# Scores of both heads made in two row groups, a ring of 30 score tiles, and the last two head pairs tested in groups of three tiles

## The reference

```python
scores = scale * np.matmul(q, k.transpose(0, 1, 3, 2))          # (2, 8, 576, 576), head_dim 64
kth = np.partition(scores, -top_k, axis=-1)[..., -top_k:-top_k + 1]   # top_k = 32
scores = np.where(scores >= kth, scores, -1000000000.0)
attn = softmax of scores along the last axis
x = np.matmul(attn, v), heads side by side                      # (1152, 512)
logits = x @ w_gate                                             # 8 experts, each token to its best
# each expert takes up to 288 tokens in order: y = relu(x @ w1[e]) @ w2[e]
out[token] = gate_w[token] * y                                  # dropped tokens stay 0
```

## Time and profile before

| | us |
|---|---|
| median of 3 runs | 535.17 (533.93 to 536.7) |
| the profiled execution, its own time | 540.3 |
| its span, first to last instruction | 538.3 |
| busy in the span: TensorE | 464.0 |
| VectorE | 308.2 |
| ScalarE | 243.7 |
| POOL | 235.8 |

### The profile page before, as it was taken

How to read it: one execution, slowest core, us unless ns; L and a number is a source line. 1 busy time by engine, 2 the same in 40 slices (tenths; PEclk the granted TensorE clock), 3 DMA queues, 4 the chain that set the end, 5 groups by cost and what they waited for, 6 DMA issues and landing times.

```text
span 538.3 us, 9099 instructions
## 1 busy us (share of the span) xinstructions
PE 464.0 (86%) x2901; PEld 390.8 (73%) x2901; DVE 308.2 (57%) x1521; ACT 243.7 (45%) x419; POOL 235.8 (44%) x197
## 2 busy tenths in 40 slices
PE   3999798899879998899797998009999999999993
PEld 2565476677656776677686886009999999999992
DVE  1699999799998999989985331300111111222222
ACT  1333685588855878567475582002131211322220
POOL 3333886587776767777756362300020210210222
PEclk9999998799987999979699698557999999999998
DMA  4111020110267240000010002479976766787400
GB/s 103 39 37 44 1 47 1 28 40 2 67 187 191 45 177 23 2 20 5 1 23 1 1 2 88 135 233 333 304 239 218 261 226 214 246 292 255 144 17 11
DMA packets 52310, 57.89 MB, mean 108 GB/s; under 512 B 33055, under 2 KB 33055, under 8 KB 52257
## 3 DMA queue, kind: packets, MB, share of 16 engines
q1 hardware_dynamic: 49984, 52.50, 31.7%
q0 software_dynamic: 2272, 4.73, 2.6%
HBM read 45.39 MB, written 14.18 MB: 111 GB/s over the span
## 4 chain that ended last, share of the span: by engine, by line
PE 38%; POOL 4%; issue 3%; DMA 3%; DVE 2%; ACT 1%; DVEq 0%; SPq 0%; POOLq 0%; ACTq 0%
PE ps_s L601 14%; PE ps_s L616 13%; PE ps_o L495 4%; PE ps_o L583 2%; PE ps_t L573 2%; PE ps_t L466 2%; POOL probs L374 2%; DMA dispatched<-x,r_slot 2%; POOL rest L369 1%; PE ps_s L506 1%; DMA scores<-dispatched 1%; PE ps_s L522 1%; POOL out_dram L407 0%; POOL dispatched L382 0%; DMA bad_row<-bad 0%
## 5 line engine op out<-in xcount | busy, mean ns | idle before, releaser
L374 POOL TENSOR_TENSOR probs<-scores,probs 128x576 f32<-128x576 f32 x72 | 101.4, 1414 | 60.8 <-ACT probs L678 58.9
L495 PE MATMUL ps_o<-v_aug,pT 128*128 128x128 f32 (+5 forms) x800 | 126.5, 300 | 0.0
L369 POOL TENSOR_TENSOR rest<-below,scores 128x576 f32<-128x576 f32 x72 | 99.9, 1408 | 55.7 <-DVE below L837 55.7
L495 PEld LDWEIGHTS ps_o<-v_aug,pT 128*128 128x128 f32 (+3 forms) x800 | 107.2, 195 | 14.5 <-issue 7.9
L449 PE MATMUL ps_s<-kT,qT 64*128 64x288 f32 x256 | 94.2, 520 | 3.5 <-ACT scores L653 2.8
L407 POOL DMA_INDIRECT out_dram<-yo,numbers x24 | 22.0, 915 | 163.5 <-DVE yo L1017 162.9
L779 DVE MAX8 cand<-scores 128x8 f32<-128x96 f32 x432 | 72.7, 240 | 17.4 <-ACT scores L653 14.9
L601 PE MATMUL ps_s<-scores,w_sb 128*128 128x192 f32 (+4 forms) x512 | 78.6, 309 | 0.6 <-ACT scores L731 0.6
L466 PE MATMUL ps_t<-ident,probs 128*128 128x128 f32 (+1 forms) x360 | 60.4, 303 | 19.7 <-ACT pT L691 15.8
L601 PEld LDWEIGHTS ps_s<-scores,w_sb 128*128 128x128 f32 x512 | 74.7, 194 | 0.9 <-ACT scores L731 0.9
L616 PE MATMUL ps_s<-scores,w_sb 128*128 128x192 f32 (+4 forms) x512 | 74.5, 304 | 0.0
(11 more groups left out here) (100 smaller groups left out, 332.4 us busy)
## 6 DMA issues: line engine op xcount, KB each, us to landing
w_sb<-in_moe_w_dram SPq DMA_DIRECT2D x16, 2048.0 KB, 9.8
dispatched<-empty SPq DMA_DIRECT2D x18, 257.0 KB, 6.3
scores<-dispatched SPq DMA_DIRECT2D x24, 192.8 KB, 3.0
out_dram<-empty SPq DMA_DIRECT2D x9, 256.0 KB, 3.1
q_nat<-in_q_dram SPq DMA_DIRECT2D x16, 128.0 KB, 2.3
k_nat<-in_k_dram SPq DMA_DIRECT2D x16, 128.0 KB, 2.4
v_aug<-in_v_dram SPq DMA_DIRECT2D x16, 128.0 KB, 2.4
out_dram<-yo,numbers POOLq DMA_INDIRECT x24, 3.4
```

The source lines that it names most:

```text
L369: nc.gpsimd.tensor_tensor(rest[:, n % 3, :], below[:, n % 3, :], score_tile(n), ALU.mult).then_inc(rest_ready, 1)
L374: nc.gpsimd.tensor_tensor(probs[:, n % PROBS, :], score_tile(n), probs[:, n % PROBS, :], ALU.subtract).then_inc(masked_ready, 1)
L495: last = nc.tensor.matmul(dst, lhs, v_aug[0:keys, g % 2, c, h, 0:width], start=(c == 0), stop=(c == TT - 1))
```

## The change

TensorE makes the scores of the two heads of a pair together, row by row (`qk_heads`): the matmuls of head 0 and head 1 alternate, head 0 into `ps_s[:, 0]` and head 1 into `ps_s[:, 1]`; the tail tile is made last (`qk_tail`). `made_at` and `tile_made` turn the order of the search into the order of making and back. The ring has 30 tiles, LEAD is 22, and w1 lies in the memory of the ring. The last two pairs are tested after every three tiles (12 tests), POOL's masks come closer from group 19 on, and the last tests stand elsewhere among VectorE's last groups. The steps of the router's work are new, and the second batch's logits have a place of their own in PSUM.

```diff
-    LEAD = 18
-    HELD = 21
-    ROUTED = [0, 2, 4, 6, 10, 12, 16]
+    LEAD = 22
+    HELD = 30
+    ROUTED = [0, 2, 4, 6, 8, 16, 19]
+    CHOSEN = 18
+    PAIRWISE = PAIRS - 2
+    CHECKS = PAIRWISE + 3 * (PAIRS - PAIRWISE)
+    ENDING = 3 * PAIRWISE
...
-        w1_sb = sb("w1_sb", [P, 2, CH, F])
...
+        w1_sb = carve(2 * CH * F).rearrange("p (u c f) -> p u c f", u=2, c=CH)
...
+        def made_at(n):
+            g, t = divmod(n, TILES)
+            return TILES * g + (2 * t if t < FULL else 2 * (t - FULL) - 1 if t > FULL else TILES - 1)
+        def tile_made(k):
+            g, e = divmod(k, TILES)
+            return TILES * g + (FULL if e == TILES - 1 else e // 2 + e % 2 * (FULL + 1))
+        def check_of(n):
+            return n // TILES if n < TILES * PAIRWISE else PAIRWISE + n // 3 - ENDING
...
-            gather_bad(6)
+            for i in range(PAIRWISE, CHECKS - 1):
+                gather_bad(i)
             load_v(7)
-            gather_bad(7)
+            gather_bad(CHECKS - 1)
...
+            masked = 0
             for m in range(GROUPS + 3):
                 if m < GROUPS:
                     push_down(3 * m)
                     push_down(3 * m + 1)
                 if m < GROUPS and m % 3 == 0:
                     push_down(3 * m + 2)
-                if m >= 3:
-                    mask(3 * (m - 3))
-                if m < GROUPS and m % 3 != 0:
+                due = 3 * (m - 2) if m <= ENDING + 2 else min(ALL, 3 * ENDING + 4 * (m - ENDING - 2))
+                if m == GROUPS + 2:
+                    due = ALL
+                for n in range(masked, due):
+                    mask(n)
+                    if n == masked and m < GROUPS and m % 3 != 0:
+                        push_down(3 * m + 2)
+                if masked >= due and m < GROUPS and m % 3 != 0:
                     push_down(3 * m + 2)
-                if m >= 3:
-                    mask(3 * (m - 3) + 1)
-                    mask(3 * (m - 3) + 2)
+                masked = max(masked, due)
...
-            def qk(n):
-                g, t = divmod(n, TILES)
-                if t == 0:
+            def qk_heads(g, r):
+                if r == 0:
                     pe.wait_ge(nat_copied, 2 * (g + 1))
-                if n >= 2:
-                    pe.wait_ge(s_ready, n - 1)
+                if g + r > 0:
+                    pe.wait_ge(s_ready, TILES * g + 2 * r)
                 for half in range(2):
                     keys = slice(half * HALF, (half + 1) * HALF)
-                    dst = ps_s[:, n % 2, half, 0:HALF]
-                    if t != FULL:
-                        h, r = (0, t) if t < FULL else (1, t - FULL - 1)
-                        last = nc.tensor.matmul(dst, qT[h * D:(h + 1) * D, g % 2, r * P:(r + 1) * P],
+                    for h in range(2):
+                        last = nc.tensor.matmul(ps_s[:, h, half, 0:HALF], qT[h * D:(h + 1) * D, g % 2, r * P:(r + 1) * P],
                                                 kT[h * D:(h + 1) * D, g % 2, keys], start=True, stop=True)
-                    else:
-                        for h in range(2):
-                            last = nc.tensor.matmul(dst[h * TAIL:(h + 1) * TAIL, :],
-                                                    qT[h * D:(h + 1) * D, g % 2, FULL * P:S],
-                                                    kT[h * D:(h + 1) * D, g % 2, keys], start=True, stop=True)
+                        if half == 1:
+                            last.then_inc(s_in_psum, 1)
...
-                    qk(s)
+                    if s % TILES == TILES - 1:
+                        qk_tail(s // TILES)
+                    elif s % TILES % 2 == 0:
+                        qk_heads(s // TILES, s % TILES // 2)
...
-                if s == ALL + ROUTED[CH] + 1:
+                if s == ALL + CHOSEN:
...
-            def copy_scores(n):
-                act.wait_ge(s_in_psum, n + 1)
+            def copy_scores(k):
+                n = tile_made(k)
+                act.wait_ge(s_in_psum, k + 1)
                 if n >= HELD:
                     act.wait_ge(masked_ready, n - HELD + 1)
+                slot = 0 if k % TILES == TILES - 1 else k % TILES % 2
                 nc.scalar.activation(score_tile(n).rearrange("p (h s) -> p h s", h=2),
-                                     ps_s[:, n % 2, :, 0:HALF], ACT.Copy, scale=SCALE).then_inc(s_ready, 1)
+                                     ps_s[:, slot, :, 0:HALF], ACT.Copy, scale=SCALE).then_inc(s_ready, 1)
...
-            def edges(g):
-                act.wait_ge(thr_checked, g + 1)
-                if g >= 2:
+            def edges(i, g, tiles):
+                act.wait_ge(thr_checked, i + 1)
+                if g >= 2 and tiles.start == 0:
                     act.wait_ge(exp_ready, TILES * (g - 1))
-                nc.scalar.activation(edge[:, g % 2, :], thr[:, g % 2, :], ACT.Copy, scale=BIG).then_inc(edges_ready, 1)
-                nc.scalar.activation(nmax[:, g % 2, :], tops[:, g % 2, :, 0], ACT.Copy, scale=-1.0).then_inc(edges_ready, 1)
+                nc.scalar.activation(edge[:, g % 2, tiles], thr[:, g % 2, tiles], ACT.Copy, scale=BIG).then_inc(edges_ready, 1)
+                nc.scalar.activation(nmax[:, g % 2, tiles], tops[:, g % 2, tiles, 0], ACT.Copy, scale=-1.0).then_inc(edges_ready, 1)
             def excess(n):
                 g, t = divmod(n, TILES)
-                if t == 0:
-                    edges(g)
-                    act.wait_ge(edges_ready, 2 * (g + 1))
+                i = check_of(n)
+                if t == 0 or i != check_of(n - 1):
+                    edges(i, g, slice(0, TILES) if g < PAIRWISE else slice(t, t + 3))
+                    act.wait_ge(edges_ready, 2 * (i + 1))
...
-                    dve.wait_ge(s_ready, n + 1)
+                    dve.wait_ge(s_ready, made_at(n) + 1)
                     after(bounded[j])
                     for c in range(SEGS):
                         part = score_tile(n)[:, c * (S // SEGS):(c + 1) * (S // SEGS)]
                         last = add(nc.vector.max(cand[:, j, c * 8:c * 8 + 8], part))
                     found.append(last)
-                    if m % 3 == 1 and m > 3 and j == 0:
-                        counted = count_bad(m // 3 - 1)
-                    if m % 3 == 1 and m > 3 and j == 1:
-                        recheck(m // 3 - 1, counted)
+                    for i in range(CHECKS):
+                        if m == (3 * i + 4 if i < PAIRWISE else i - PAIRWISE + ENDING + 2):
+                            if j == 0:
+                                counted = count_bad(i)
+                            if j == 1:
+                                recheck(i, counted)
...
+            def tiles_of(i):
+                return (i, slice(0, TILES)) if i < PAIRWISE else (i // 3 + PAIRWISE * 2 // 3, slice(i % 3 * 3, i % 3 * 3 + 3))
...
+                if m == GROUPS:
+                    recheck(CHECKS - 2, count_bad(CHECKS - 2))
                 if m > 0:
                     search_rest(m - 1)
                     pick(m - 1)
-                if m > 0 and m % 3 == 0:
+                if m > 0 and m % 3 == 0 and m <= ENDING:
                     find_bad(m // 3 - 1)
+                if m > ENDING:
+                    find_bad(m - 1 - ENDING + PAIRWISE)
                 if m < GROUPS:
                     mark_below(m)
-            recheck(PAIRS - 1, count_bad(PAIRS - 1))
+            normalise(PAIRS - 2, 0)
+            recheck(CHECKS - 1, count_bad(CHECKS - 1))
             dve.wait_ge(consts_ready, 11)
-            normalise(PAIRS - 2, 0)
             choose_experts(0)
             normalise(PAIRS - 2, 1)
             assign_slots(0)
```

44 lines of the change are left out of this document (27 added, 17 removed).

## The result

The change made the kernel **slower by 1.4%**: 542.23 us, the median of 14 runs (539.49 to 545.35), against 535.6 for the kernel before, run beside it on the same chip (14 runs, 529.53 to 542.52). The ratio is 1.014, 95% interval 1.0107 to 1.0172. The ratios leave out executions over 1.5% above the fastest of their kernel (4 of the kernel before here, none of the changed one); by the medians of all it is 1.2%, and the ratios of the first four experiments lie 0.4 to 0.9% above those of their medians, mostly for the same reason. I had forecast 525.7 us, a range of 516 to 534, and faster with a chance of 0.81: the time lies outside the range, and it moved the other way.

A forecast was written before the change was run, and what follows sets the result against it. It took VectorE to pace the search, with TensorE working off a late tail and then the experts. Terms 5.5 - 2.0 + 1.6 + 1.0 - 15.6 = -9.5 us, from the 535.17 median, gave 525.7 us, range 516 to 534.

The forecast's parts named there:

- start, third group of tiles: At the start, pairs of tiles wait for both score copies; VectorE's third group at 41.0 against 35.48: +5.5 us, nothing absorbs it.
- wait for the row of counts: On SP's queue, the last pair's v load behind one more gather lands before its first user: nothing.
- more tests: On VectorE, 12 tests instead of 8, about 0.4 us each: +1.6 us for four.
- `picked`: In the last groups, POOL's masks sit next to `picked` more often, up to two more collisions: +1.0 us, bounds 0 and 2.8.
- tail: After E, the last test frees three tiles instead of nine; attention ends at E + 32.2 instead of E + 47.8: -15.6 us.
- LEAD and HELD: In the search, VectorE's first three waits for weighted values stay, the fourth, 2.03 us, goes: -2.0 us.
- fourth rival: TensorE goes cold behind every test; normalisation waits after all seven, +11.4, slow tail +5.1: +7, 542 us; chance 0.1.
- a slow tail: After the last test, TensorE runs 10.3 us at half speed, costing 5.1; as a rival 533 us, chance 0.13.
- the clock did not come early: Rival: 2.4 GHz already in the first stage, start costs 1.5, 521.7 us; or the waits go, 515.9; chance 0.2.
- The scores: On TensorE, two tiles together cost some 1.2 us; 34 us less work over 64 tiles, counted as nothing in the search.

The follow-up runs named there:

- the first four experiments: Against the changed kernel: gather of test 6 ahead of pair 6's v load, 533.14 us; LEAD 23, 531.75; both, 524.73; scores one head at a time, 546.04.
- gather first: The changed kernel, but SP gathers the counts of test 6 ahead of the v load of head pair 6: 533.14 us, 0.9991.
- the fastest version: The changed kernel with LEAD 22, test 6's gather ahead of pair 6's v load, and next pair's q and k transposed one step earlier: 518.7 us, 0.9658.
- the version with both edits: The changed kernel with the gather of test 6 ahead of the v load and LEAD 23 instead of 22: 524.73 us, 0.9847.

## Why the prediction was wrong

What I forecast and what the trace has, up to E (from the two first traces):

| term | forecast | measured |
|---|---|---|
| start, third group of tiles | +5.5 | +5.2 |
| waits for weighted values in the search | -2.0 | +6.1 (7.8 to 13.9) |
| wait for the row of counts | 0 | +4.7 (a group of 16.7 us instead of 12.0) |
| more tests | +1.6 | not separable; the rest leaves +1.6 |
| `picked` (26.0 us in all before) | +1.0 | -3.2 (22.8) |
| E | +6.1 | +14.4 |
| tail | -15.6 | -12.1 |

The two traces are 0.3 us apart, where I had summed up -9.5: 9.2 us are missing. The other 7 us between 525.7 and 542.23 are no term of the sum. I took the sum from a median although its rows came from an execution 5 us over it, and the changed kernel's trace lies 2 us under its own.

- **The step that failed** is the one on LEAD and HELD: "the four waits of VectorE depend on the same three or four steps after a test", from which I took 0 for the first three, with bounds of -5.8 and +8.4. They aren't the same steps. I had the rule by which ScalarE stops, s = 9g + LEAD, and the rule by which q and k are transposed, s mod 9 = 4, and didn't set 22 mod 9 beside it. What the runs show in its place: with the transposition one step away, on either side of the stop, the waits are gone (lead of 23; transposition at t = 3), and so with a lead of 18; with it at the stop they are 13.8 us (gather first) or 13.9 (the change). What it needs beside the line is the clock's fall. Moving the transposition gave 16.4 us of median time; in the traces with the gather first E moved by 13.6, of which 3.6 came before VectorE's sixth group, at the start and at the first stop. The bound of +8.4 doesn't fit my own fourth rival, which puts the same case at +11.4; measured was +8.1 up to the fourth of the new waits, against the 5.8 that I kept.
- **A missing term**: of SP's queue I looked at the v load of the last pair, which stands behind a gather. The load of pair 6 stands ahead of one. It waits for TensorE, and with it VectorE waited 4.95 us; I had put this term at nothing. Alone it cost 9.1 us (the waits behind the tests kept) or 7.1 (without them).
- **The slower rival** had the right place, waits behind tests (four, not seven), at a chance of 0.1. Its time of 542 is the measured one by luck: its waits were to cost 11.4 us more and a slow tail 5.1, the waits cost 8.1 and the tail missed by 3.6, and the wait for the counts it doesn't have. Its mechanism was half of it: the clock did fall behind five tests, but with the transposition moved the same lead and the same pairing fall to 1.2 GHz for 3.4 to 6.8 us about the tests as well, and nothing waits. That the steps are shorter by their scores, its argument against itself, is borne out (heads apart: 546.04 us).
- **The start** was right in size, third group at 40.65 against a forecast of 41.0, and the clock did not come early: eight records took 2.29 us there. "Nothing absorbs it" holds up to the sixth group (+7.2 in the changed kernel, +3.3 in the fastest). What it leaves out is that the lead of 22 costs there by itself: with the first pair one head at a time the sixth group comes no earlier (68.45 against 68.66). And with a lead of 18 the loss is gone by E (281.6 with pairs, 282.3 with the heads apart).
- **The scores** overlap as forecast, and that TensorE's shorter work is hidden in the search is borne out by the pair of kernels with a lead of 18, 529.68 and 529.62 us.
- **The tail**: the last test was over at 308.9, E + 11.8 (forecast 10.7). VectorE's choice of experts then took 5.3 us instead of 4.7, so that TensorE's wait for the ranking ended at E + 17.3 (forecast 15.4); it took 2.23 us. What stands behind it took 18.4 us instead of 16.8, with the clock at half from 314.2 to 317.6. Without that, in the version with both edits, it took 17.0 us. VectorE of the changed kernel (0.95 us for `r_before` in the earlier trace rows), and TensorE:

```profile
307.61 0.27 DVE L890 TENSOR_REDUCE worst<-bad_row 1x1 int32<-1x128 f32 x1 [1.16 <-DMA bad_row<-bad]
...
312.19 2.07 DVE L967 TENSOR_TENSOR r_before<-r_before,r_hot 128x8 bf16<-128x8 bf16 x5
```

```profile
314.37 0.21 PE L559 MATMUL ps_s<-r_hot,tri 128*128 128x40 bf16 x1 [2.23 <-DVEq L968]
...
314.47 1.30 PE L494 MATMUL ps_t<-ident,probs 128*128 128x128 f32 x5
```

- **The `picked` collisions** went the other way, 22.8 us instead of 26.0. They shift with every edit (21.7 to 27.8 us in all over the versions), and I had no row for its sign.

Against the sum the fastest version stands like this: I forecast 530.8 us for a traced execution, and its trace took 518.7. E is at 276.8 instead of 288.8, the tail 34.3 us instead of 32.2. Of the 12.0 us at E, 5.8 are the waits that I had kept (none is left, the lower bound that I named) and 2.2 the start; the rest isn't separated. What follows the attention took 2.1 us less than in the kernel before, within the spread of that kernel's traces.

## What to carry to other kernels

When a depth of software pipelining is changed, every step at which an engine stops is shifted against all periodic work that is keyed to the step: write down the residue of each stop and of each periodic item (here 22 mod 9 = 4 against t = 4), and look at what stands in line behind each stop, on each in-order queue. For a queue that only issues transfers, read every load that stands ahead of a small urgent transfer, and what that load waits for. And a wait that starts with an idle TensorE is paid twice, since the work it releases may run at the lower clock: look for serial steps ahead of the released work before blaming the clock, since here moving them took the waits away though the clock still fell.

## What the runs showed of the hardware

- Two row groups, each writing all 128 columns into its own PSUM bank, ran side by side in float32: 1.24 us for eight records against 1.13 for four.
- The scores of the first pairs ran at 2.29 us for eight records, against 1.24 later; TensorE had work for some two thirds of that time (2.29 of 3.56 us). In the version with both edits the granted clock is recorded as 0.50 from 25.3 to 73.1. The changed kernel's trace records no clock before 75.3, where a window reads as 1.00; the time of the records is the better sign there.
- A removed wait of 4.95 us was worth 9.1 us of median time, 7.7 between the traces. In three of the traces that have that wait (the changed kernel, lead of 23, transposition moved alone) the clock falls three times between it and the end of the attention; in three without it (gather first, both edits, the fastest) once or never. With the heads apart, though, it falls once behind a wait of 7.64 us, for 10.3 us. So the link is open.
- TensorE's filler work of 4.15 us in each of four gaps gained 6.4 us by the medians against the same kernel without it (526.73 against 533.14, of different rounds).
